# Fill matmuls in two more pauses of the routing, and another order on VectorE in the second-last expert tile

## The chip, the cores and the metric

One NeuronCore of a Trainium2 chip runs the whole program in one launch. The metric is the device time of one execution in microseconds; three runs of the kernel before gave 856.67, 857.29 and 859.13, with a median of 857.29.

## The reference

Three stages follow each other, all in float32.

- Attention with pooled queries: 16 heads (2 batches of 8) of 1152 keys and 64 columns; pairs of queries are averaged, so there are 576 queries for each head; softmax over the keys, product with the values. The result is laid out as x, 1152 tokens of 512 columns.
- A mixture of experts: x goes through two small products with w_gate and w_noise, from which noisy logits for 8 experts follow. Each token takes its best two experts, with softmax weights of these two, and gets the weighted sum of relu(x @ w1[e]) @ w2[e], with 1024 hidden columns.
- A dense layer: h = x @ w_in (2048 columns), g = h * cos(h), out = g @ w_out.

```python
logits = x @ w_gate
noisy_logits = logits + np.log1p(np.exp(x @ w_noise)) * noise
top2 = np.argpartition(-noisy_logits, 2, axis=1)[:, :2]
...
h = np.maximum(x[mask] @ w1[e], 0.0)
out[mask] += top2_w[mask, k, None] * (h @ w2[e])
...
h = x @ w_in
return (h * np.cos(h)) @ w_out
```

## The kernel before, in words

The program is written engine by engine: each engine has its own instruction stream, in the order of the code, and waits for semaphores that others raise. Nothing is scheduled by a planner. Large products are made of three matmuls in fp32r: each operand is split into a high part and a low part (the rest), and high x high, high x low and low x high are summed in PSUM (`split_product`, L1633 to L1635). So each operand needs a high half (a copy on ScalarE, `hh` in L862) and a low half (a subtraction on VectorE, `hl` in L1293, in `low_h`).

The attention runs to about 308 us. Its last step on TensorE is `turn_o` for the last head (L1470): ScalarE copies the head's output out of PSUM (L747, semaphore `ot_ev`), and TensorE turns it.

The routing follows, 308 to 326 us, with TensorE and VectorE in turns. VectorE makes noisy logits, the best two, and running counts by a scan (`upto`, L1113). TensorE makes ranks from them (`rank_of`, L1510 to L1514), and each expert's first tokens are picked by matmuls with a selection matrix (`first_tile`, L1527; once for each batch; VectorE makes the matrix `sel` in L1118 from `mine` in L1117). A table says which token stands in which slot (L1624, 20 matmuls of 26 columns); the gathers of x on GpSimd wait for it. `warm(n)` issues n matmuls of 512 columns on weights that lie in SBUF, into a PSUM bank that nobody reads (`IDLE`, bank 7; L1520). The kernel before calls it twice with WARM_R = 4: after the second ranks, and after the second `first_tile`. TensorE waits for `w_ready` (the weights of expert 0 are split) ahead of the second `rank_of`.

Then 25 expert tiles of 128 slots each. For tile t, TensorE turns the hidden values (`turn_h`, L1672), computes `hidden(t + 1)`, turns x for t + 2 (`turn_x`, L1648; not in the last tiles), and computes `expert_out(t)`, which waits for both low halves (`hl_ev` at 2t + 2). On VectorE, `tile_steps(t)` issues `low_h(t)`, `relu_d(t + 1)` (half of the ReLU, L1288), `low_x(t + 2)` and `move_y(t)` (L1300). `left` counts the tiles left after this one: in tile 23 `left` is 1, in tile 24 it is 0.

The first three token tiles of the dense layer are put together during the last two expert tiles. For slots of tiles up to 22, rows are gathered from DRAM by GpSimd, scaled by ScalarE (L886) and added by VectorE (`add_second`, L1307). For slots of tiles 23 and 24, `late_rows` (L1689) on TensorE multiplies the output tile by a selection matrix of gates, `late_sel`. VectorE prepares all this in `late_tiles()` at the start of tile 23: places and slot numbers (L1312 to L1319, semaphore `rt2_done`, for which GpSimd's gathers wait), and the gates (L1324 and L1327, for each of the two late tiles).

Of the kernel before, what the change touches and what calls it, by code (L numbers as in the profile page):

```python
# [10 lines left out]
ALU = mybir.AluOpType  # L11
# [4 lines left out]
P = 128  # L16
BANK = 512
# [25 lines left out]
WPIECES = 4  # L43
# [46 lines left out]
def bank_of(hh, slot):  # L90

    return 6 + (TURNS.index(slot) + hh) % 2
# [27 lines left out]
def build(nc, q, k, v, w_gate, w_noise, noise, w1, w2, w_in, w_out, out, x_rows, x_slots, y_slots, route):  # L120
    ctx = ExitStack()
    with ctx:
        def sem(name):
            return ctx.enter_context(nc.semaphore(name))
# [72 lines left out]
        w_ready = sem("w_ready")  # L197
# [53 lines left out]
        ps = ctx.enter_context(nc.psum_tensor("ps", [P, 8, BANK], F32))  # L251
        RANK0, RANK1, COUNTS, TABLE, IDLE = 7, 4, 5, 6, 7
# [15 lines left out]
        def place(name, at, shape, dt=F32):  # L268
            size = 4
            for n in shape[1:]:  # L270
                size *= n
            return nc.alloc_sbuf_tensor_at(name, shape, dt, offset=base + at), -(-(at + size) // 32) * 32


        W, at = place("W", 0, [P, 2, 2, 2 * DM * F // P], F32R)
# [26 lines left out]
        late_slot, at = place("late_slot", at, [P, 2])  # L302
# [96 lines left out]
        rtb, at = place("rtb", XD + 10240, [P, BLK, 4])  # L399
        late_sel, at = place("late_sel", at, [P, 2, BLK])  # L400
        assert at <= REGION + REGION_BYTES
        late_n, at = place("late_n", REGION + BLK_T * 2 * DM * 4, [P, 2, BLK])
# [576 lines left out]
        def _(dve):  # L979
            ve = nc.vector  # L980
            step_count = [0]

            def then(ins):

                step_count[0] += 1
                ins.then_inc(dve_step, 1)
                dve.wait_ge(dve_step, step_count[0])
# [246 lines left out]
            for n in range(2):  # L1234
                last = ve.tensor_tensor(based[:, n, :, :], onehot[:, n, :, :],
                                        tbase[:, :].unsqueeze(2).to_broadcast([P, E, RT]), ALU.mult)
            then(last)
            for n in range(2):
                last = ve.tensor_reduce(tile_of[:, n, :], based[:, n, :, :].rearrange("p e i -> p i e"), AX_X, ALU.add)
# [7 lines left out]
            last = ve.tensor_tensor(late[:, :, :], cum[0:1, 0:E - 1].unsqueeze(1).to_broadcast([1, SLOTS_T, E - 1]),  # L1247
                             iota_t[0:1, 0:SLOTS_T].unsqueeze(2).to_broadcast([1, SLOTS_T, E - 1]), ALU.is_le)
# [12 lines left out]
            def low_w(j):  # L1261

                dve.wait_ge(wh_done, WPIECES + j + 1)
                part = slice(j * WPIECE, (j + 1) * WPIECE)
                ve.tensor_tensor(W[:, 1, 1, part], stage[:, j % 2, :], W[:, 1, 0, part].bitcast(F32), ALU.subtract
                                 ).then_inc(w_ready, 1)

            def low_out(j):

                dve.wait_ge(oh_done, j + 1)  # L1270
                ve.tensor_tensor(W[:, 1, 1, j * WPIECE:(j + 1) * WPIECE], stage[:, j % 2, :],
                                 W[:, 1, 0, j * WPIECE:(j + 1) * WPIECE].bitcast(F32), ALU.subtract).then_inc(ol_done, 1)
# [9 lines left out]
            def low_x(t):  # L1282
                dve.wait_ge(xh_ev, t + 1)
                ve.tensor_tensor(xl[:, :, :], x_turned(t), xh[:, :, :].bitcast(F32), ALU.subtract).then_inc(xl_ev, 1)

            def relu_d(t):
                dve.wait_ge(h_done, 2 * t + 2)
                ve.tensor_scalar(hid[:, BANK:F], ps[:, 1, :], 0.0, None, ALU.max).then_inc(hid_d, 1)  # L1288

            def low_h(t):  # L1290
                for n in range(2):
                    dve.wait_ge(hh_ev, 2 * t + n + 1)
                    ve.tensor_tensor(hl[:, 4 * n:4 * n + 4, :].rearrange("p c n -> p (c n)"), ps[:, 2 + n, :],  # L1293
                                     hh[:, 4 * n:4 * n + 4, :].rearrange("p c n -> p (c n)").bitcast(F32),
                                     ALU.subtract).then_inc(hl_ev, 1)

            def move_y(t):
                dve.wait_ge(y_done, t + 2)
                at_least(dve, y_stored, 16 * t)
                ve.tensor_copy(ys[:, :], ps[:, 5, :]).then_inc(y_ev, 1)  # L1300

            def add_second(i):
                dve.wait_ge(xa_done, i + 1)
                dve.wait_ge(second_in[i % BLK_T], 16 * (i // BLK_T + 1))
                first = yg[:, i % BLK_T, 0, :]
                gate = gate_on[:, i, 1:2] if i < BLK_T else rt2[:, i, 3:4]
                ve.scalar_tensor_tensor(first, yg[:, i % BLK_T, 1, :], gate, first, ALU.mult, ALU.add).then_inc(x2_done, 1)  # L1307

            def late_tiles():

                dve.wait_ge(rt_loaded, 16)
                then(ve.scalar_tensor_tensor(pos_on[:, :, :], rt2[:, 0:BLK_T, 0:2], float(LATE * P), rt2[:, 0:BLK_T, 0:2],  # L1312
                                             ALU.is_lt, ALU.mult))
                ve.scalar_tensor_tensor(gate_on[:, :, :], rt2[:, 0:BLK_T, 0:2], float(LATE * P), rt2[:, 0:BLK_T, 2:4],
                                        ALU.is_lt, ALU.mult)
                ve.tensor_copy(pos2_u[:, BLK_T:TT, :], rt2[:, BLK_T:TT, 0:2])
                ve.tensor_copy(pos2_u[:, 0:BLK_T, :], pos_on[:, :, :]).then_inc(rt2_done, 1)
                for k in range(2):
                    last = ve.tensor_scalar(late_slot[:, k:k + 1], tok[:, 0:1], float((LATE + k) * P), None, ALU.add)  # L1319
                then(last)  # L1320
                dve.wait_ge(rtb_loaded, 16)
                for k in range(2):
                    for n in range(2):
                        last = ve.scalar_tensor_tensor(late_n[:, n, :], rtb[:, :, n], late_slot[:, k:k + 1], rtb[:, :, 2 + n],  # L1324
                                                       ALU.is_equal, ALU.mult)
                    then(last)
                    then(ve.tensor_tensor(late_sel[:, k, :], late_n[:, 0, :], late_n[:, 1, :], ALU.add))  # L1327

            def tile_steps(t, left=3, first=False):
                if left == 1:  # L1330
                    late_tiles()
                low_h(t)
                if left == 0:
                    add_second(1)
                    add_second(2)
                    low_out(0)
                    low_out(1)
                if first:
                    low_w(2)
                if left >= 1:  # L1340
                    relu_d(t + 1)
                if left == 1:
                    add_second(0)
                if first:
                    low_w(3)
                if left >= 2:
                    low_x(t + 2)
                move_y(t)
# [7 lines left out]
            relu_d(0)  # L1356
            low_x(1)
            tile_steps(0, first=True)
            with dve.Fori(1, SLOTS_T - 2) as t:
                tile_steps(t)  # L1360
            for left in (1, 0):
                tile_steps(SLOTS_T - 1 - left, left=left)
# [49 lines left out]
        def _(pe):  # L1412
# [53 lines left out]
            def turn_o(p, hh):  # L1466
                g = 2 * p + hh
                pe.wait_ge(ot_ev, g + 1)
                for c in range(QC):
                    last = pe.matmul(ps[:, bank_of(hh, ("o", 0)), c * TURN:(c + 1) * TURN], ot[0:D + 1, c * P:(c + 1) * P],  # L1470
                                     turner[:, bass.ds(g, 1), :].rearrange("p o n -> p (o n)"), start=True, stop=True)
                last.then_inc(ot_done, 1)
# [41 lines left out]
                    pe.matmul(ps[:, COUNTS, 0:E], ones[:, :], upto[:, :, RT - 1], start=True, stop=True  # L1514
                              ).then_inc(rank_done, 1)

            def warm(n):

                for i in range(n):
                    pe.matmul(ps[:, IDLE, :], W[:, 0, 0, 0:P], W[:, 0, 0, 0:BANK], start=True, stop=True)  # L1520

            def first_tile(b, sel):

# [58 lines left out]
            for c in range(QC):  # L1582

                at_least(pe, m0_ev, c - 1)
                for a in range(3):
                    last = pe.matmul(ps[:, 2 + c % 2 * 3 + a, 0:PIECE], qat[:, 0, c * P:(c + 1) * P],
                                     kt[:, 0, a * PIECE:(a + 1) * PIECE], start=True, stop=True)
# [20 lines left out]
            products(NHEAD // 2 - 1, 2, KC - 1)  # L1608
            pe.wait_ge(o_norm, NHEAD - 1)
            pe.wait_ge(rank_read, 1)  # L1610
            turn_o(NHEAD // 2 - 1, 1)


            first_tile(0, sel0)
            pe.wait_ge(w_ready, WPIECES)
            rank_of(1, RANK1)
            warm(WARM_R)
            first_tile(1, sel1)
            warm(WARM_R)
            pe.wait_ge(slot_of_done, 1)  # L1620
            pe.wait_ge(rows_done, 2)
            for n in range(2):
                for i in range(RT):
                    last = pe.matmul(ps[:, TABLE, 0:STW], row_of[:, n, i, :], tile_hot[:, n, i, :],  # L1624
                                     start=(n + i == 0), stop=(n * RT + i == 2 * RT - 1))
# [177 lines left out]
```

## Time and profile before

| | |
|---|---|
| three runs, us | 856.67, 857.29, 859.13 (median 857.29) |
| profiled execution, us | 856.61 |
| its span, from the first to the last instruction, us | 854.9 |
| TensorE (PE) busy | 838.0 us, 98% of the span |
| VectorE (DVE) busy | 499.9 us, 58% |
| ScalarE (ACT) busy | 421.9 us, 49% |
| GpSimd (POOL) busy | 402.1 us, 47% |
| mean granted TensorE clock | 0.998 |

The profiled execution's own time is 1.7 us over its span. PE's busy time goes by modelled ends of pipelined matmuls, so that the starts of instructions are the surer reading. A granted clock of 1.00 is 2.4 GHz, 0.50 is 1.2 GHz. "Idle before" is the time in which an engine stood, with the instruction that released it; "issue" stands where the profile shows no releaser.

### The profile page before, as it was taken

The page shows a single profiled execution, that of the slowest core. Times are in us where ns is not written, and L with a number is a line of the kernel's source. Part 1 is how long each engine was busy: PE and PEld are TensorE (multiplying, and loading weights), DVE is VectorE, ACT ScalarE, POOL GpSimd, SP SyncE. Part 2 cuts the span into 40 slices and gives each one's busy share as a digit, 9 for nine tenths or more (in the row PEclk, how much of TensorE's full clock was granted, in tenths as well). Part 3 has the DMA queues.
Part 4 walks back from the last instruction along what each step waited for, and adds up shares of the span by engine and source line. Part 5 has one row for each costly group of instructions (what it writes and reads, how often), then busy time and mean ns, then how long its engine had stood idle before and what let it go on. Part 6 is the DMA issues. An engine that isn't in the chain of part 4 may idle for free.

```text
span 854.9 us, 15389 instructions
## 1 busy us (share of the span) xinstructions
PE 838.0 (98%) x4860; PEld 744.4 (87%) x4861; DVE 499.9 (58%) x995; ACT 421.9 (49%) x776; POOL 402.1 (47%) x293
## 2 busy tenths in 40 slices
PE   7999999999999989999999999999999999999998
PEld 6899999999999887888887888888878889999897
DVE  7788877888778886423232322232266776676664
ACT  3777777777777763212111211121144665464554
POOL 7554445555877104649859959577422030000000
PEclk9999999999999999999999999999999999999999
DMA  5212211142242015986645545353444020000100
GB/s 132 66 43 62 64 41 41 41 141 73 94 128 95 1 56 188 305 307 224 236 155 176 193 146 184 130 201 133 137 130 154 1 74 19 20 0 1 38 1 37
DMA packets 51520, 91.27 MB, mean 107 GB/s; under 512 B 9376, under 2 KB 18592, under 8 KB 50976
## 3 DMA queue, kind: packets, MB, share of 16 engines
q1 hardware_dynamic: 40832, 67.26, 23.4%
q10 hardware_dynamic: 7296, 12.59, 4.5%
q0 software_dynamic: 3360, 11.01, 4.4%
q8 instruction: 18, 0.29, 0.1%
q14 instruction: 14, 0.11, 0.0%
HBM read 73.78 MB, written 17.06 MB: 106 GB/s over the span
## 4 chain that ended last, share of the span: by engine, by line
PE 90%; DVE 5%; ACT 2%; POOL 2%; issue 1%; DMA 0%; DVEq 0%; POOLq 0%; ACTq 0%
PE ps L1633 10%; PE ps L1635 10%; PE ps L1634 10%; PE ps L1455 5%; PE ps L1485 5%; PE ps L1501 4%; PE ps L1503 4%; PE ps L1502 4%; PE ps L1486 4%; PE ps L1760 4%; PE ps L1759 3%; PE ps L1758 3%; PE ps L1745 3%; PE ps L1743 3%; PE ps L1744 3%; PE ps L1672 2%
## 5 line engine op out<-in xcount | busy, mean ns | idle before, releaser
L639 POOL TENSOR_TENSOR W<-stage,W 128x2048 fp32r<-128x2048 f32 x32 | 147.1, 4598 | 2.6
L1023 DVE TENSOR_REDUCE mx<-ps 128x1 f32<-128x384 f32 x225 | 119.5, 550 | 17.3 <-PE ps L1455 17.3
L1035 DVE TENSOR_TENSOR pl__80<-ps,ph 128x576 fp32r<-128x576 f32 x144 | 107.9, 750 | 33.4 <-ACT ps L793 33.4
L788 ACT ACTIVATE ph<-ps 128x576 fp32r<-128x576 f32 x144 | 93.9, 652 | 53.5 <-PE ps L1486 52.5
L793 ACT ACTIVATE ps<-ps 128x576 f32<-128x576 f32 x144 | 93.4, 649 | 0.0
L862 ACT CAST hh<-ps 128x512 fp32r<-128x512 f32 x50 | 26.9, 590 | 124.2 <-PE ps L1672 113.5
L1501 PE MATMUL ps<-ph,vs 128*65 128x288 f32 x288 | 86.0, 299 | 0.4 <-ACT ot L747 0.4
L1485 PE MATMUL ps<-qat,kt 128*128 128x288 f32 x288 | 83.8, 306 | 1.3 <-DVE tok L1198 0.6
L1503 PE MATMUL ps<-ph,vs 128*65 128x288 f32 x288 | 84.7, 294 | 0.0
L1502 PE MATMUL ps<-pl__80,vs 128*65 128x288 f32 x288 | 84.6, 294 | 0.0
L1633 PE MATMUL ps<-W,xh 128*128 (+1 forms) x200 | 80.8, 404 | 1.0 <-POOL W L639 0.7
L1633 PE MATMUL ps<-W,hh 128*128 (+1 forms) x200 | 80.1, 401 | 1.3 <-issue 1.3
L1486 PE MATMUL ps<-qbt,k 128*128 128x288 f32 x288 | 80.3, 294 | 0.0
L1635 PE MATMUL ps<-W,xl 128*128 (+1 forms) x200 | 78.6, 393 | 0.0
L1634 PE MATMUL ps<-W,xh 128*128 (+1 forms) x200 | 78.5, 393 | 0.0
L1635 PE MATMUL ps<-W,hl 128*128 (+1 forms) x200 | 78.2, 391 | 0.0
L1634 PE MATMUL ps<-W,hh 128*128 (+1 forms) x200 | 78.0, 390 | 0.0
L1455 PE MATMUL ps<-kt,qat 128*128 128x384 f32 x225 | 76.1, 352 | 1.7 <-ACT qat L727 0.9
L1300 DVE COPY ys<-ps 128x512 f32<-128x512 f32 x25 | 17.3, 692 | 101.2 <-PE ps L1635 101.2
L1288 DVE TENSOR_SCALAR hid<-ps 128x512 f32<-128x512 f32 x25 | 17.3, 691 | 91.9 <-PE ps L1635 91.9
L1743 PE MATMUL ps<-fh,W 128*128 128x384 f32 x192 | 64.9, 338 | 0.0
L1745 PE MATMUL ps<-fh,W 128*128 128x384 f32 x192 | 64.8, 337 | 0.0
(220 smaller groups left out, 1959.3 us busy)
## 6 DMA issues: line engine op xcount, KB each, us to landing
stage<-in_moe_w_dram SPq DMA_DIRECT2D x32, 1024.0 KB, 5.5
y_slots<-ys ACTq DMA_DIRECT2D x25, 256.0 KB, 2.0
x_slots<-ring SPq DMA_DIRECT2D x22, 256.0 KB, 3.8
xs<-x_slots ACTq DMA_DIRECT2D x22, 256.0 KB, 2.7
kn<-in_k_dram SPq DMA_DIRECT2D x16, 288.0 KB, 3.4
vn<-in_v_dram SPq DMA_DIRECT2D x16, 288.0 KB, 2.9
stage<-in_moe_w_in_dram SPq DMA_DIRECT2D x4, 1024.0 KB, 5.0
stage<-in_moe_w_out_dram SPq DMA_DIRECT2D x4, 1024.0 KB, 5.7
```

Of the source, the lines that this page charges most:

```text
L639: pl.tensor_tensor(W[:, slot, 1, part], stage[:, j % 2, :], W[:, slot, 0, part].bitcast(F32), ALU.subtract).then_inc(w_ready, 1)
L1023: ve.tensor_reduce(mx3[:, i:i + 1], ps[:, bank_of(hh, ("m", i)), 0:PIECE], AX_X, ALU.max).then_inc(m_ev, 1)
L1035: ve.tensor_tensor(pl_[:, j % 3, :].rearrange("p (a n) -> p a n", a=2), ps[:, 2 * s_par(hh, j):2 * s_par(hh, j) + 2, 0:HQ], ph[:, j % 3, : ...
L1455: pe.matmul(ps[:, bank_of(hh, ("m", i)), 0:PIECE], qat[:, par, c * P:(c + 1) * P], kt[:, par, a * PIECE:(a + 1) * PIECE], start=True, stop ...
L1485: pe.matmul(ps[:, 2 * sp_ + a, 0:HQ], kt[:, par, keys], qat[:, par, cols], start=True, stop=False)
L1486: last = pe.matmul(ps[:, 2 * sp_ + a, 0:HQ], k1[:, par, keys], qbt[:, par, cols], start=False, stop=True)
L1501: pe.matmul(dst, vs[:, par, j, 0, :], ph[:, j % 3, cols], start=(j == 0), stop=False)
L1502: pe.matmul(dst, vs[:, par, j, 0, :], pl_[:, j % 3, cols], start=False, stop=False)
L1503: last = pe.matmul(dst, vs[:, par, j, 1, :], ph[:, j % 3, cols], start=False, stop=(j == KC - 1))
L1633: pe.matmul(dst, hi, rhs_of(i, 0), start=(i == 0), stop=False)
L1634: pe.matmul(dst, hi, rhs_of(i, 1), start=False, stop=False)
L1635: last = pe.matmul(dst, lo, rhs_of(i, 0), start=False, stop=(i == n - 1))
```

## The change

On VectorE, `late_tiles` becomes two functions, `late_places` and `late_gates(k)`. The places stay ahead of `low_h(23)`; the gates of the first late tile come behind `low_h(23)`, those of the second behind `relu_d(24)`. On TensorE, `warm` takes a bank, and is called twice more: three matmuls into bank 7 ahead of the last `turn_o`, and five into bank 5 behind the first `first_tile`. The wait for `w_ready` moves ahead of the first of them.

```diff
-            def late_tiles():
+            def late_places():
...
+            def late_gates(k):
+
                 dve.wait_ge(rtb_loaded, 16)
-                for k in range(2):
-                    for n in range(2):
-                        last = ve.scalar_tensor_tensor(late_n[:, n, :], rtb[:, :, n], late_slot[:, k:k + 1], rtb[:, :, 2 + n],
-                                                       ALU.is_equal, ALU.mult)
-                    then(last)
-                    then(ve.tensor_tensor(late_sel[:, k, :], late_n[:, 0, :], late_n[:, 1, :], ALU.add))
+                for n in range(2):
+                    last = ve.scalar_tensor_tensor(late_n[:, n, :], rtb[:, :, n], late_slot[:, k:k + 1], rtb[:, :, 2 + n],
+                                                   ALU.is_equal, ALU.mult)
+                then(last)
+                then(ve.tensor_tensor(late_sel[:, k, :], late_n[:, 0, :], late_n[:, 1, :], ALU.add))
 
             def tile_steps(t, left=3, first=False):
                 if left == 1:
-                    late_tiles()
+                    late_places()
                 low_h(t)
+                if left == 1:
+                    late_gates(0)
                 if left == 0:
                     add_second(1)
                     add_second(2)
@@
                 if left >= 1:
                     relu_d(t + 1)
                 if left == 1:
+                    late_gates(1)
                     add_second(0)
@@
-            def warm(n):
+            def warm(n, bank=IDLE):
 
                 for i in range(n):
-                    pe.matmul(ps[:, IDLE, :], W[:, 0, 0, 0:P], W[:, 0, 0, 0:BANK], start=True, stop=True)
+                    pe.matmul(ps[:, bank, :], W[:, 0, 0, 0:P], W[:, 0, 0, 0:BANK], start=True, stop=True)
@@
             pe.wait_ge(o_norm, NHEAD - 1)
             pe.wait_ge(rank_read, 1)
+            pe.wait_ge(w_ready, WPIECES)
+            warm(3, 7)
             turn_o(NHEAD // 2 - 1, 1)
 
 
             first_tile(0, sel0)
-            pe.wait_ge(w_ready, WPIECES)
+            warm(5, 5)
             rank_of(1, RANK1)
             warm(WARM_R)
             first_tile(1, sel1)
```

## Rows read from the trace of the kernel before

**Rows 1.** The page's chain of work that ended last, share of the span by engine.

```profile
PE 90%; DVE 5%; ACT 2%; POOL 2%; issue 1%; DMA 0%; DVEq 0%; POOLq 0%; ACTq 0%
```

**Rows 2.** Windows: length, busy us of each engine (instructions), granted clock, DMA, GB/s.

```profile
290.00:326.00 36.00, 32.94 (x253) 30.48 (x251) 28.62 (x126) 24.86 (x51) 0.00 (x0) 1.00 0.10 34
326.00:327.00 1.00, 1.00 (x7) 1.00 (x7) 0.26 (x3) 0.00 (x0) 0.00 (x0) 0.72 0.00 0
327.00:330.00 3.00, 3.00 (x9) 2.28 (x9) 2.93 (x6) 0.00 (x0) 2.48 (x2) 0.52 0.30 81
```

**Rows 3.** PE timeline, first hidden tile: start, us, line, tile, count [idle before <-releaser].

```profile
326.55 0.78 PE L1633 MATMUL ps<-W,xh 128*128 128x512 f32 x1
327.12 0.63 PE L1634 MATMUL ps<-W,xh 128*128 128x512 f32 x1
327.55 0.63 PE L1635 MATMUL ps<-W,xl 128*128 128x512 f32 x1
...
330.00 0.39 PE L1635 MATMUL ps<-W,xl 128*128 128x512 f32 x1
330.22 0.39 PE L1633 MATMUL ps<-W,xh 128*128 128x512 f32 x1
```

**Rows 4.** PE timeline, the routing.

```profile
308.05 0.29 PE L1503 MATMUL ps<-ph,vs 128*65 128x288 f32 x1
309.16 1.31 PE L1470 MATMUL ps<-turner,ot 65*128 65x81 f32 x10 [0.82 <-ACT ot L747]
310.31 4.67 PE L1527 MATMUL ps<-sel,x 128*128 128x128 f32 x40
316.15 0.39 PE L1510 MATMUL ps<-member,tri 128*128 128x40 f32 x2 [1.18 <-DVE upto L1113]
316.37 0.39 PE L1511 MATMUL ps<-upto,ones 128*128 128x40 f32 x2
...
316.82 1.18 PE L1520 MATMUL ps<-W 128*128 128x512 f32 x4
318.26 4.73 PE L1527 MATMUL ps<-sel,x 128*128 128x128 f32 x40 [0.27 <-DVE sel L1118]
...
324.27 2.44 PE L1624 MATMUL ps<-tile_hot,row_of 128*128 128x26 f32 x20 [0.35 <-ACT row_of L827]
```

**Rows 5.** Timelines of ScalarE, VectorE and GpSimd in the routing.

```profile
308.38 0.63 ACT L747 COPY ot<-ps 65x576 f32<-65x576 f32 x1 [2.26 <-PE ps L1503]
...
310.57 0.17 DVE L1046 TENSOR_SCALAR den_o<-ps 128x5 f32<-128x5 f32 x1 [0.31 <-DVE place_f L1134]
...
317.19 0.16 DVE L1117 SCALAR_TENSOR_TENSOR mine<-ps,member 128x5 f32<-128x5 f32 x1
...
327.22 1.12 POOL L673 DMA_INDIRECT xd<-x_rows,tok_u  x1 [46.95 <-DVE tok_u L1352]
```

**Rows 6.** ScalarE timeline, second high half of tile 23.

```profile
619.18 0.59 ACT L862 CAST hh<-ps 128x512 fp32r<-128x512 f32 x1
```

**Rows 7.** PE timeline, hidden(24), expert_out(23) and late_rows(0).

```profile
624.16 0.39 PE L1635 MATMUL ps<-W,xl 128*128 x1
625.87 0.50 PE L1633 MATMUL ps<-W,hh 128*128 x1 [1.31 <-issue]
...
632.38 2.85 PE L1689 MATMUL ps<-late_sel,ys 128*128 128x384 f32 x8
```

**Rows 8.** VectorE timeline, tile 23 and the start of tile 24.

```profile
619.62 1.71 DVE L1324 SCALAR_TENSOR_TENSOR late_n<-rtb,late_slot 128x384 f32<-128x384 f32 x2
621.37 0.56 DVE L1327 TENSOR_TENSOR late_sel<-late_n 128x384 f32<-128x384 f32 x1
...
624.31 1.29 DVE L1293 TENSOR_TENSOR hl<-ps,hh 128x512 fp32r<-128x512 f32 x2
625.51 0.68 DVE L1288 TENSOR_SCALAR hid<-ps 128x512 f32<-128x512 f32 x1
626.89 0.75 DVE L1307 SCALAR_TENSOR_TENSOR yg<-yg,gate_on 128x512 f32<-128x512 f32 x1 [0.69 <-DMA yg<-y_slots,pos_u]
631.63 0.69 DVE L1300 COPY ys<-ps 128x512 f32<-128x512 f32 x1 [3.99 <-PE ps L1635]
```

## The prediction

> **What bounds the kernel now.** I read the chain that ended last first: TensorE holds 90% of it and VectorE 5% [rows 1], so the end moves only by what TensorE itself is spared or made to wait. Then the granted clock by stretches: it is 1.00 over the whole routing (290 to 326 us), 0.72 in the microsecond after it, 0.52 in the next three. With a mean of 0.998 over 854.9 us (0.002 x 854.9 = 1.7 us of full clock missing, or 3.4 us at half) this is the one low stretch of the execution [rows 2]. Then TensorE's own timeline. At the low level (0.5 of full, so 1.2 GHz) one product of 512 columns follows another after 0.43 us, at the high level (2.4 GHz) after 0.23 us. From 326.55 to 330.00 us eight products are started in 3.45 us where 8 x 0.23 = 1.84 would do, so the low stretch costs 1.6 us [rows 3]. Last, TensorE's pauses. In the routing there are three small ones: 0.82 us before the turn of the last head (L1470), released by ScalarE's copy, 1.18 us before the ranks (L1510), released by VectorE's scan, and 0.3 us before the second selection [rows 4, 5]. In the last expert tiles there is one: the last product of hidden(24) starts at 624.16, the first of expert_out(23) only at 625.87, after 1.31 us of idle [rows 7]. The releaser is given as "issue", so I looked for it on VectorE. There the two low halves (L1293) of tile 23 run from 624.31 for 1.29 us, up to 625.60, directly before TensorE goes on; ScalarE's second high half had been there since 619.18 + 0.59 = 619.77 [rows 6, 8]. What stands before the low halves on VectorE are the gates of the two late tiles: two groups of 1.71 us and 0.56 us each. This wait is for hl_ev, and the gates make it.
>
> **Part 1, last expert tiles (VectorE).** Nothing is added or removed: four multiply-compares and two additions keep their forms. Before, the gates ran from 619.62 to about 624.27. After, the low halves start where the gates did or slightly earlier, limited by the high halves: the second is in at 619.77, so the low halves end by 619.8 + 1.29 = 621.1 at the latest. TensorE gets to expert_out(23) at 624.16 + 0.23 = 624.39, so 3.3 us of slack: the wait is gone. The idle time says 1.31 us; the starts say more, 625.87 - 624.39 = 1.48. The idle time goes by a modelled end of the last matmul, and the starts are what shifts the work behind them. I take 1.5 and keep 1.3 as the lower end.
>
> What is late next? Gates 0 (1.71 + 0.03 + 0.56 + 0.04 = 2.34 us) now stand ahead of the ReLU of tile 24 (L1288): 621.1 + 2.34 = 623.4, while the ReLU needs the end of hidden(24), 624.16 + 0.39 = 624.55. 1.1 us of cover. If that cover were gone, it would still cost nothing: the reader of the ReLU stands behind the 24 products of expert_out(23), 24 x 0.23 = 5.5 us. So the ReLU runs at 624.6 to 625.3, 0.9 earlier than its 625.51. Gates 1 then take up to 627.6, and the first add_second (L1307), at 626.89 now, moves to 627.6 and ends at 628.4. Behind it VectorE waits for the copy of tile 23's output, at 631.63 now and at 630.1 with the gain, 1.7 us later [rows 8]. The readers of the gates, late_rows at 632.38 now, come at 630.9, 3.3 us after gates 1 [rows 7]. The gathers are started from the places, which stay ahead of the low halves, so POOL's queue and its transfers keep their times. SP's queue is passed by nothing. All further work hangs on TensorE's chain and moves as a whole: -1.5 us.
>
> **Part 2, the two pauses (TensorE).** Added: 3 + 5 = 8 matmuls of 512 columns with their weight loads, into banks 7 and 5 whose old contents are read by then. The wait for the first weights (w_ready) moves ahead of the turn of the last head, with the fill, the turn and the whole selection queued behind it; but POOL has had nothing to do for 46.95 us before 327.22 us, so that all of its splits were done by 280.3 and this wait costs nothing [rows 5].
> Three in the first pause: TensorE's input is free at 308.05 + 0.13 = 308.18; the existing four take 1.18 us, so three take 1.18 - 0.23 = 0.95 with the last one's drain, 0.2 less until the input is free: 308.95. The turn starts at 309.16 now, being released by ScalarE's copy (308.38 + 0.63 = 309.01) [rows 4, 5]. Cost 0. Upper end: with the drain the fills reach to 308.2 + 0.95 = 309.15, and a wait's latency more makes the turn 0.1 late. Lower end -0.1, if an engine that streams starts the turn sooner than one that stood. This place has no cover: the turn heads VectorE's chain from 310.57 on.
> Five in the second: 1.18 + 0.23 = 1.41 with drain from 314.85, so 316.05 to 316.26 against 316.15 now; 0.1 late at most. The ranks (L1510, L1511, over at 316.37 + 0.39 = 316.76) have their reader, L1117 on VectorE, at 317.19, because VectorE still builds rows. 0.4 us of cover. Cost 0. If the cover were gone, it would be 0.1. The four fills and the second selection behind (318.26) have 0.27 us to spare [rows 4, 5].
> What does it bring? By the rows of this execution nothing fell in or after these pauses: the clock is 1.00 up to 326 us [rows 2]. What stands before the fall at about 326.5 is the table (L1624): 20 matmuls of 26 columns in 2.44 us, TensorE "busy" all along [rows 4]. The new fills lie 8 and 15 us earlier, with dense work, 4.7 us of selection and four fills, in between. I take 0 for the clock; the other end is -1.6, the whole low stretch gone. If it went, hidden(0) would end 1.6 us sooner, at 332.3; tile 1's gather, started at 327.22, has 5 us by then.
>
> The Trainium skill (TensorE: Matmul & The Clock Gate, "HAM oscillation — how this bites in real kernels") puts the fall of the clock down to long idle gaps between bursts of matmuls. Neither filled pause (0.8 and 1.2 us) is such a gap, and the trace agrees in that the clock stays at 1.00 through both; it disagrees in that the fall here follows an unbroken run of narrow matmuls. By the page the fills bring 0, as in my sum.
>
> **Sum.** Against the profiled execution: span 854.9, 1.7 around it, 856.61 in all; -1.5 + 0 + 0 = 855.1. The median of the runs before is 857.29, 0.7 above the profiled one, and the slowest, 859.13, is 2.5 above: about one low stretch more. I put the step on the median: 857.29 - 1.5 = 855.8.
>
> **Rivals.** A: *the low stretch goes.* For it: several pauses and narrow matmuls from 308 to 326 lie close together, and the fall may answer to this whole sparse stretch, not to the table alone; the spread of the runs suggests that stretches come and go between executions. Against: the table itself is untouched. 857.29 - 1.5 - 1.6 = 854.2.
> B: *the wait at 624 us is not hl's, or another comes as late.* For it: the profile names no releaser. Against: low halves and restart lie 0.26 us apart, and every other tile runs through without gap. -0.0: 857.3. Half of it would be 856.5.
> C: *slower.* The clock falls before the fills, in the pause at 308 us, and the fills run at 0.43 us each ahead of waiting work. Three take 1.3 us from 308.18: turn 0.35 late. The selection behind it loses up to 1.65 us of its pause of 1.18, 0.5 late; the five fills take 2.15 instead of 1.2, and the ranks twice their 0.6, which less the cover of 0.4 makes 1.0 late. In sum 1.85 against 1.5: 857.6. It decides from 1.5 us of delay. For it: the spread of the runs; against it: clock 1.00 there in the only trace.
> D: *the fills do more than the profiled execution can show*, since in the slower executions the clock falls after one of these pauses: the median comes down to the profiled one less 1.5, 855.1.
>
> **How the numbers follow.** Forecast (855.8, own range 855.2 to 856.6) 0.50; D 0.13; A 0.22; B 0.10; C 0.05. What a measurement of this kernel can tell from no change is about 0.3%, 2.6 us, so faster means under 854.7. That is A, and a tail of D and the forecast: 0.22 + 0.05 = 0.27. Slower means over 859.9: C at its worst, 0.03. The rest, 0.70, is within. Range: from just below A, 853.9, to B with the noise of the runs, 857.5.
>
> **What would show it.** Part 1 right: no idle before L1633 near 624 us, expert_out(23) starting 0.23 us after the last product of hidden(24), low halves done by 621.2, and the ReLU of tile 24 waiting for TensorE. Part 1 wrong: an idle time of over 0.3 us there, or a new one before L1672 or L1689. Part 2 right: fills end before 309.2 and 316.3, L1117 on VectorE not later against the turn, and the products of hidden(0) again 0.43 us apart for some 3 us. If they are 0.23 apart from the first on, A holds. If fills are 0.43 apart, C. A median under 854.7 or over 857.5 makes the prediction wrong.

## The result, and the profile after

The changed kernel has a median of 854.89 us (20 runs, 853.63 to 856.67); the kernel before, run beside it 20 times, 858.07. The ratio is 0.9965, 95% interval 0.9951 to 0.9978: 3.0 us less. A second set, run later with the last experiments (12 runs beside 23 of before), gave 0.9974 (0.9954 to 0.9994), 2.2 us less. The profiled execution took 854.54 us, its span is 852.8, 2.1 us under the one of before; its mean granted clock is 1.000, where it was 0.998.

The page's span, and the chain of work that ended last by engine. The chain has the same shape as before; TensorE's share is 89% where it was 90%:

```profile
span 852.8 us, 15404 instructions
PE 89%; DVE 5%; ACT 2%; issue 2%; POOL 2%; DMA 0%; DVEq 0%; POOLq 0%; ACTq 0%
```

The windows that answer to [rows 2]. The granted clock is the third figure from the end of a row:

```profile
290.00:326.00 36.00, 34.86 (x262) 31.85 (x260) 28.59 (x126) 24.71 (x50) 0.00 (x0) 1.00 0.10 34
326.00:327.00 1.00, 1.00 (x7) 0.91 (x7) 0.52 (x4) 0.00 (x0) 0.08 (x1) 1.00 0.00 0
327.00:330.00 3.00, 3.00 (x14) 2.44 (x13) 2.97 (x4) 0.60 (x1) 2.69 (x2) 1.00 0.30 87
```

The clock stays at 2.4 GHz where it had been at 1.2: 14 matmuls in the last window instead of 9. TensorE's timeline of the routing, for [rows 3 and 4] (L1475 is the turn, L1525 the fills, L1515 the ranks, L1631 the table, L1640 the first product of a group):

```profile
308.01 0.85 PE L1525 MATMUL ps<-W 128*128 128x512 f32 x3
308.90 1.34 PE L1475 MATMUL ps<-turner,ot 65*128 65x81 f32 x10
...
314.50 1.39 PE L1525 MATMUL ps<-W 128*128 128x512 f32 x5
315.83 0.42 PE L1515 MATMUL ps<-member,tri 128*128 128x40 f32 x2
...
324.04 2.37 PE L1631 MATMUL ps<-tile_hot,row_of 128*128 128x26 f32 x20 [0.35 <-ACT row_of L827]
326.26 0.48 PE L1640 MATMUL ps<-W,xh 128*128 128x512 f32 x1
326.58 0.39 PE L1641 MATMUL ps<-W,xh 128*128 128x512 f32 x1
```

And ScalarE's copy and the two places of VectorE, for [rows 5]:

```profile
308.21 0.64 ACT L747 COPY ot<-ps 65x576 f32<-65x576 f32 x1 [2.25 <-PE ps L1508]
...
310.34 0.17 DVE L1046 TENSOR_SCALAR den_o<-ps 128x5 f32<-128x5 f32 x1 [0.25 <-DVE place_f L1134]
...
316.96 0.16 DVE L1117 SCALAR_TENSOR_TENSOR mine<-ps,member 128x5 f32<-128x5 f32 x1
```

Both pauses are filled and neither chain waits: the turn starts 0.05 us after the copy (over at 308.21 + 0.64 = 308.85), where it was 0.15 before (309.01 to 309.16 [rows 4, 5]), and VectorE's L1117 starts 6.62 us after L1046, as before (317.19 - 310.57). From there to the table nothing moved either.

Tile 23 on TensorE and VectorE, for [rows 7 and 8] (gates are L1326 and L1329 now):

```profile
623.78 0.39 PE L1642 MATMUL ps<-W,xl 128*128 x1
624.01 0.39 PE L1640 MATMUL ps<-W,hh 128*128 x1
...
630.40 2.85 PE L1696 MATMUL ps<-late_sel,ys 128*128 128x384 f32 x8
```

```profile
619.21 1.29 DVE L1293 TENSOR_TENSOR hl<-ps,hh 128x512 fp32r<-128x512 f32 x2
620.42 1.72 DVE L1326 SCALAR_TENSOR_TENSOR late_n<-rtb,late_slot 128x384 f32<-128x384 f32 x2
622.17 0.56 DVE L1329 TENSOR_TENSOR late_sel<-late_n 128x384 f32<-128x384 f32 x1
624.28 0.69 DVE L1288 TENSOR_SCALAR hid<-ps 128x512 f32<-128x512 f32 x1 [1.55 <-PE ps L1642]
624.89 1.70 DVE L1326 SCALAR_TENSOR_TENSOR late_n<-rtb,late_slot 128x384 f32<-128x384 f32 x2
...
627.33 0.75 DVE L1307 SCALAR_TENSOR_TENSOR yg<-yg,gate_on 128x512 f32<-128x512 f32 x1
629.65 0.69 DVE L1300 COPY ys<-ps 128x512 f32<-128x512 f32 x1 [1.57 <-PE ps L1642]
```

The idle time is gone: the next group follows after 0.23 us. From the turns of tile 23 to those of tile 24 it is 11.80 us where it was 13.37.

**Where 2.1 us came from.** I followed the start of each tile's turns of the hidden values (L1672 before, L1679 after). hidden(0) starts 0.3 us earlier (326.26 for 326.55), 0.2 of it from ahead of the routing and 0.1 from the turn. Tile 0's turns start 1.83 us earlier (332.86 for 334.69): the low stretch is gone, worth 1.55. But tile 23's turns start only 0.41 us earlier (617.65 for 618.06). 1.4 us were given back on the way, 0.64 of them between tiles 1 and 2. VectorE and TensorE there, after:

```profile
343.94 2.29 DVE L1265 TENSOR_TENSOR W<-stage,W 128x2048 fp32r<-128x2048 f32 x1 [3.33 <-issue]
346.15 0.68 DVE L1284 TENSOR_TENSOR xl<-ps,xh 128x512 fp32r<-128x512 f32 x1
...
347.04 0.50 PE L1640 MATMUL ps<-W,xh 128*128 x1 [0.36 <-DVE xl L1284]
```

The last piece of expert 1's weights (L1265) is paced by its load, and it is queued ahead of the low half of x for tile 2 (L1284). Its high half on ScalarE waits for the transfer:

```profile
342.00 1.91 ACT L834 CAST W<-stage 128x2048 fp32r<-128x2048 f32 x1 [4.87 <-DMA stage<-in_moe_w_dram]
```

In the kernel before, this piece and the low half behind it came at the same times (343.82 and 346.03), and nobody waited, since TensorE itself was 1.8 us later. The rest, 0.8 us, comes from the pace of the tiles: 12.29 us each where it was 12.25, over 21 tiles. Here the turns of three tiles after the change (starts 12.30 and 12.29 apart):

```profile
383.12 1.03 PE L1679 MATMUL ps<-ident,hid 128*128 128x128 f32 x8
395.42 1.03 PE L1679 MATMUL ps<-ident,hid 128*128 128x128 f32 x8
407.71 1.03 PE L1679 MATMUL ps<-ident,hid 128*128 128x128 f32 x8
```

Then tile 23 adds 1.57. In sum 0.3 + 1.55 - 0.64 - 0.8 + 1.57 = 2.0, and 0.1 behind tile 24. The 0.8 us of the pace are not the change's doing, as the last section shows; without them this pair of profiles would lie 2.9 us apart.

### The profile page after: what moved, and what is told of

It is laid out like the page before. It is cut to its first block, busy times and chain, and to the rows that moved or that the text cites. A ratio compares the mean times of both kernels' runs of the same rounds, so it can differ in the third digit from the quotient of the medians.

```text
span 852.8 us, 15404 instructions
## 1 busy us (share of the span) xinstructions
PE 838.9 (98%) x4868; PEld 744.4 (87%) x4869; DVE 499.0 (59%) x995; ACT 422.2 (50%) x776; POOL 402.5 (47%) x293
## 4 chain that ended last, share of the span: by engine, by line
PE 89%; DVE 5%; ACT 2%; issue 2%; POOL 2%; DMA 0%; DVEq 0%; POOLq 0%; ACTq 0%
PE ps L1640 10%; PE ps L1642 10%; PE ps L1641 10%; PE ps L1460 5%; PE ps L1490 5%; PE ps L1506 4%; PE ps L1508 4%; PE ps L1507 4%; PE ps L1491 4%; PE ps L1766 4%; PE ps L1767 4%; PE ps L1765 4%; PE ps L1752 3%; PE ps L1750 3%; PE ps L1751 3%; PE ps L1679 2%
## 5 line engine op out<-in xcount | busy, mean ns | idle before, releaser
L1640 PE MATMUL ps<-W,xh 128*128 (+1 forms) x200 | 80.4, 402 | 1.3 <-POOL W L639 0.7
L1640 PE MATMUL ps<-W,hh 128*128 (+1 forms) x200 | 80.4, 402 | 0.0
```

The lines of the kernel that those rows point to most:

```text
L1640: pe.matmul(dst, hi, rhs_of(i, 0), start=(i == 0), stop=False)
```

## The experiments

Eleven runs: ten further kernels, and the changed one again. Medians differ from set to set, so each ratio is against the runs of the kernel before on the same chip, and each number of microseconds is worked out from the ratio. The mean granted clock of an execution tells how many low stretches it had behind its start: one of them takes it down by 0.002, as in [rows 2]. Over the three chips of the experiments the kernel before ran 90 times: 17 times without one, 48 times with one, 25 with two; by a line through these runs one stretch is worth 1.2 us. That is a rough figure: on the single chips the line gives 0.8, 1.2 and 1.6 us, and on the one of the wide table the few executions without a stretch were no faster than those with one (857.7 and 857.4 us on average). In the profiles a stretch in the start costs 1.2 to 1.4 us: from the turns of qb to the copy of the last head it is 293.3 to 293.5 us with it and 292.1 without. One at 326 us costs 1.55.

One thing the granted clock does not show is how long TensorE stays slow at the very start. The same six matmuls in the profile of before:

```profile
8.85 1.31 PE L1586 MATMUL ps<-kt,qat 128*128 128x384 f32 x6 [0.67 <-ACT qat L727]
```

And in the second profile of the changed kernel, with its window:

```profile
10.03 2.29 PE L1591 MATMUL ps<-kt,qat 128*128 128x384 f32 x6 [0.68 <-ACT qat L727]
...
8.00:12.00 4.00, 3.33 (x13) 2.92 (x12) 1.10 (x2) 1.51 (x4) 2.42 (x3) 1.00 0.81 178
```

In the second, they take 2.29 us for 1.31, and the slower pace lasts to about 15 us under a granted clock of 1.00; the last head's copy starts 2.6 us later (310.94 for 308.38). Over the thirteen profiles the turns of qb start anywhere from 16.0 to 18.9 us, and of all the edits only the fills of the start, in the last kernel, touch anything near them. So a time is more than its count of low stretches.

**Each edit alone, and each pause alone.** The order alone leaves both calls of the fills out, and the wait for `w_ready` is back in its old place (so too in each kernel below without the first fills):

```diff
-            warm(3, 7)
...
-            warm(5, 5)
```

> The new order on VectorE alone, no fills. Theory (each edit has its own share): 1.5 us of idle before expert_out(23) goes, nothing else, so about -1.5 against the kernel before (ratio 0.998), and low stretches of the clock in the routing as before. Rival (the order is all): ratio 0.9965 as with both edits. Rival (the fills are all): ratio 1.000.

Ratio 0.9983 (0.9972 to 0.9993), 1.46 us less; 1.1 low stretches an execution, as before. In its profile the stretch at 326 us is there, and the turns of tile 24 follow those of tile 23 after 11.78 us, where it was 13.37. This is the first theory's number.

The fills alone put both gates ahead of the low halves again:

```diff
                 if left == 1:
                     late_places()
+                    late_gates(0)
+                    late_gates(1)
                 low_h(t)
-                if left == 1:
-                    late_gates(0)
...
                 if left == 1:
-                    late_gates(1)
                     add_second(0)
```

> The fills alone, all gates ahead of the low halves again. Theory: the idle time of about 1.3 to 1.5 us before expert_out(23) is back, and what the two edits gave together beyond the order's share stays: about -1.3 (ratio 0.9985), since low stretches become fewer over the executions. Rival (the fills do nothing and the profiled execution was lucky): ratio 1.000, mean granted clocks as in the kernel before.

Ratio 0.9994 (0.9981 to 1.0007): 0.5 us less, unclear, and under the 1.3 that I expected. But the clock did move: 7 of 11 executions had no low stretch, where 5 of 33 of the kernel before on this chip had none; on average 0.36 for 1.1. The idle time is back:

```profile
628.09 0.50 PE L1639 MATMUL ps<-W,hh 128*128 x1 [1.28 <-issue]
```

Its profiled execution shows a second place where the clock falls, the start of the kernel; three other profiles show it too, the one with the fills of the first pause alone and the two with the wide table and no fills. This is the window in question:

```profile
24.00:26.00 2.00, 2.00 (x10) 1.86 (x9) 1.96 (x5) 1.19 (x2) 1.86 (x3) 0.50 0.03 8
```

Then one pause at a time, with the new order:

> Both edits less the five fills of the second pause: three fills ahead of the last turn_o stay. If the first pause matters for the clock and the second does not: as with both edits, ratio 0.9965. If it is the second that matters: as the order alone, 0.998. If they add up: 0.997 to 0.9975.

> Both edits less the three fills of the first pause: five fills ahead of the second ranks stay. If the second pause (1.18 us, the longer one) is what lets the clock fall: ratio 0.9965. If it is the first: as the order alone, 0.998. Either way the place costs nothing to TensorE's successors: L1117 on VectorE does not wait.

Three fills in the first pause: 0.9977 (0.9966 to 0.9988). Five in the second: 0.9984 (0.9973 to 0.9996). Neither can be told from the order alone by its time. By the clock they have 1.0 low stretch an execution each, with one execution of 11 without any, as the order alone. Both fills together gave the 0.36 above on the same chip. The changed kernel, with the same fills, has 0.7 over both its sets (11 of 32 without any), but in the second of them 0.75 beside 0.83 of the kernel before, 4 of 12 without any beside 9 of 23. So one fill alone did nothing that these runs can tell, both together helped clearly on one chip and not on another, and which of them saves which stretch is not settled.

**What lets the clock fall.** The table's matmuls have 26 columns, and I took them to be paced by their weight loads, so I let each stream its columns eight times:

```diff
-                    last = pe.matmul(ps[:, TABLE, 0:STW], row_of[:, n, i, :], tile_hot[:, n, i, :],
+                    last = pe.matmul(ps[:, TABLE, 0:WIDE * STW], row_of[:, n, i, :],
+                                     tile_hot[:, n, i, :].unsqueeze(1).to_broadcast([P, WIDE, STW]),
```

> Both edits, and each of the 20 matmuls of the table streams its 26 columns eight times (208 columns into the same bank, the first 26 are read), so the array has work behind each weight load. Theory (narrow matmuls of the table let the clock fall): no low stretch at 326 us in any execution, table still about 2.4 us since the weight loads pace it, hidden(0) at 0.23 us a product. Time against both edits: the stretch is worth 1.6 us on TensorE, of which 0.6 is given back at hidden(2), so where it had been, -1.0; over all executions about -0.4. Rival (the fall answers to the whole routing): the stretch stays in about half of the executions and the time is that of both edits, ratio 0.9965 to 0.998. Rival (208 columns cost time of their own): table over 2.6 us.

Ratio 0.9962 (0.9948 to 0.9977), by its time not to be told from the changed kernel. 9 of 12 executions had no low stretch, 0.25 on average; I had expected none in any. The table costs what it did, within 0.1 us, so its own columns do not pace it:

```profile
324.23 2.47 PE L1632 MATMUL ps<-tile_hot,row_of 128*128 128x208 f32 x20 [0.36 <-ACT row_of L828]
```

Its low half of x for tile 2 waits as after the change. The next kernel takes that wait away by an order on VectorE, and the same on ScalarE (`high_w(3)` behind `move_x`):

```diff
-                if first:
-                    low_w(3)
                 if left >= 2:
                     low_x(t + 2)
+                if first:
+                    low_w(3)
```

> As the run with the wide table, and in tile 0 the last piece of expert 1's weights (high part on ScalarE, low part on VectorE) comes behind the x of tile 2 on both engines. Theory: with the clock up, hidden(2) stands 0.4 to 0.6 us for the low half of x, which is queued behind this piece, and this wait goes: 0.4 to 0.6 us less than the wide table alone. Rival (the x of tile 2 is late for itself, by its gather): no change there.

Ratio 0.9956 (0.9941 to 0.9972), the lowest ratio of all; against the wide table alone 0.5 us less, within the intervals. The mechanism shows in the profile: the low half of x is 5.2 us earlier, the last weight piece comes behind it, and tile 2's turns follow tile 1's after 12.25 us instead of 12.89.

```profile
340.94 0.69 DVE L1286 TENSOR_TENSOR xl<-ps,xh 128x512 fp32r<-128x512 f32 x1 [0.36 <-ACT xh L851]
345.24 2.29 DVE L1267 TENSOR_TENSOR W<-stage,W 128x2048 fp32r<-128x2048 f32 x1 [3.61 <-ACT W L835]
```

The wide table in the kernel before, and with the other two but no fills:

> The kernel before with the wide table alone: no fills in the pauses, gates ahead of the low halves. Theory (the table is what lets the clock fall at 326 us): low stretch there gone, ratio 0.999, all else as before. If the pauses matter besides: some executions keep a low stretch. It also tells about the tile loop: products of a tile took 12.25 us from turn to turn where the execution had a low stretch at 326 us and 12.29 where it had none. If this follows the clock, it is 12.29 here; if it follows the fills of the first pause (the place of the loop in the code), 12.25.

> No fills in the two pauses; new order in tile 23, wide table, x of tile 2 ahead of the last weight piece. Theory: the fills are not needed once the table is wide; time as with both edits and these two (ratio 0.996). Rival (both fills keep the clock up besides): low stretches in a larger share of the executions and 0.5 to 1 us more than with the fills.

The table alone gave 0.9980 (0.9967 to 0.9993), 1.7 us less by the ratio, though the medians are only 0.8 apart (856.87 and 857.68). It has 0.33 low stretches an execution where the kernel before has 1.25 on this chip, and 8 of 12 executions without any for 3 of 34; this is what shows that the narrow table matters to the clock. Without the fills but with all else it was 0.9965 (0.9951 to 0.9978), with 0.36 low stretches; that is 0.8 us over the 0.9956 with the fills, but the intervals overlap, so what the fills bring beside the wide table is not decided. Both profiles have a low stretch that no other profile has, behind the unfilled second pause. Windows and selection of the kernel before with the wide table (clock third from the end):

```profile
319.00:323.00 4.00, 3.75 (x20) 3.62 (x20) 3.65 (x20) 3.01 (x6) 0.00 (x0) 0.57 0.00 0
```

```profile
317.28 0.39 PE L1511 MATMUL ps<-member,tri 128*128 128x40 f32 x2 [1.18 <-DVE upto L1114]
...
319.39 6.23 PE L1528 MATMUL ps<-sel,x 128*128 128x128 f32 x40 [0.25 <-DVE sel L1119]
```

The second selection takes 6.23 us for 4.73 [rows 4]. So the clock can fall behind this pause, and in the profiled execution of before it did not. Of the five profiles without fills in the second pause these two show it; of the seven with fills in both pauses none does. That speaks for the pause as the cause, but so few profiles do not show it, and both also had a stretch in the start.

**The costs of the fills.** Both doubled, `warm(6, 7)` and `warm(10, 5)`:

> Both fills doubled: six ahead of the last turn_o, ten behind the first selection. It tests the costs of the sum. Theory: three and five just fit. Three more cost 3 x 0.23 = 0.7 us at turn_o, with no cover. Five more end 1.15 us later; the ranks then end 0.75 us after L1117 on VectorE could start, as the cover is 0.4. In sum the table comes about 1.4 us later than with both edits. Rival (the fills are hidden further, since VectorE and ScalarE set the pace of the routing): table later by under 0.5 us.

A single execution, for its profile (856.85 us; its start was slow, with the turns of qb at 18.19 us for 16.11, so this time says nothing on the fills):

```profile
310.08 1.53 PE L1525 MATMUL ps<-W 128*128 128x512 f32 x6
311.45 1.24 PE L1475 MATMUL ps<-turner,ot 65*128 65x81 f32 x10
...
316.95 2.55 PE L1525 MATMUL ps<-W 128*128 128x512 f32 x10
319.34 0.31 PE L1515 MATMUL ps<-member,tri 128*128 128x40 f32 x2
```

```profile
319.90 0.16 DVE L1117 SCALAR_TENSOR_TENSOR mine<-ps,member 128x5 f32<-128x5 f32 x1 [0.41 <-PE ps L1516]
```

The turn starts 0.53 us after the copy (310.92) instead of 0.05, and L1117 waits 0.41 us. From the copy to the table 16.1 us instead of 15.2: 0.9 us in all, between my 1.4 and the rival's 0.5. The sizes three and five fit; doubled, the first makes the turn 0.5 us later and the second makes L1117 wait 0.4.

**The changed kernel again, and the start.** The last kernel adds to the one with the wide table and x first

```diff
             qb_group(0, 0, 1)
+            warm_up(WARM_S)
...
+                                if early and hh == 1 and i == 0:
+                                    warm_up(WARM_S + 2)
                                 max_scores(p, hh, i)
```

where `warm_up(n)` issues n matmuls of 384 columns into bank 5, and WARM_S is 3.

> Both edits, wide table, x of tile 2 first, and fills of 384 columns in two pauses of the start as well: three before the first scores of head 0 (pause of 0.6 us), five before the first maxima of head 1 (pause of 0.9 us). Theory (a low stretch falls where pauses crowd, and one such place is 16 to 24 us): the stretch seen at 23.6 us in two of the profiles goes, mean clock near 1.000, and the median 0.3 to 0.5 us under the version without these fills. Rival (fills in the start delay the scores or maxima): first turn_o later by 0.2 us or more, and nothing won.

> The changed kernel once more, beside the others on one chip. As a yardstick: ratio 0.9965 to 0.9975, about two thirds of a low stretch an execution, and the version with the wide table and x first 0.5 to 1 us under it. Its tile pace may be 12.25 or 12.29 us: if it is 12.25 here, the pace belongs to the execution and not to the kernel.

On one chip: the changed kernel 855.18 us (0.9974, 0.9954 to 0.9994), with 0.75 low stretches; the one with all of it 853.94 (0.9960, 0.9944 to 0.9976), and 11 of 12 executions without any. Its median is the lowest of all, but its ratio is not (0.9956 without the fills of the start, on another chip, with 8 of 12 executions without a stretch). The two were not run side by side, so what these fills add is not shown. They fit the first pause: the scores start 1.56 us after the turns of qb (16.91 to 18.47), as in the kernel before (16.31 to 17.87).

```profile
17.62 0.77 PE L1533 MATMUL ps<-kt,qat 128*128 128x384 f32 x3
18.47 0.37 PE L1493 MATMUL ps<-qat,kt 128*128 128x288 f32 x1
...
19.44 1.12 PE L1533 MATMUL ps<-kt,qat 128*128 128x384 f32 x5
20.53 0.62 PE L1463 MATMUL ps<-kt,qat 128*128 128x384 f32 x2
```

And the pace: the same changed kernel, which had 12.29 us a tile in its first profile, has 12.26 and 12.25 here. The low stretch behind the table is there again in this profile:

```profile
386.80 1.03 PE L1679 MATMUL ps<-ident,hid 128*128 128x128 f32 x8
399.06 1.03 PE L1679 MATMUL ps<-ident,hid 128*128 128x128 f32 x8
411.31 0.93 PE L1679 MATMUL ps<-ident,hid 128*128 128x128 f32 x7
```

## Why the prediction was right, and where not

The time, 854.89 us, lies in the stated range (853.9 to 857.5), but not in the forecast's own (855.2 to 856.6), and is nearest to rival D's 855.1. The step was forecast as 1.5 us and measured as 3.0 and 2.2. So the range held by its rivals, and only the first part of the sum held by its mechanism.

**Part 1 was right in place and size.** 1.5 us was forecast; the profile gives 1.57 (13.37 less 11.80), the order alone 1.46 by its ratio. The wait was hl_ev's. The low halves ended at 620.50 (forecast 621.1), the ReLU started at 624.28 (624.6) with TensorE as its releaser, gates 1 ended at 627.18 (627.6), and none of the moved work made anyone wait. The fills alone brought the idle time back. Rival B is out.

**Part 2 was right in its costs, wrong in what it brings.** Cost 0, with bounds of 0.1 on either side: the turn starts 0.1 us sooner after the copy, the lower end. The term that was mis-sized is the clock's. The step that failed is "by the rows of this execution nothing fell in or after these pauses", from which I took 0. It is true of that execution and was no ground for the median: the clock's falls differ between executions of one kernel, and a profile shows one. The kernel before had 1.1 low stretches an execution (0.8 to 1.25 by chip). Its own profile shows one behind the table; two more places, the start and behind the second pause, are seen in profiles of kernels that have its code there. The changed one has 0.7. At 1.2 us a stretch that is 0.5 us, as an estimate; in the changed kernel's second set it is 0.75 beside 0.83, or 0.1 us. By times, the share of the fills is 0.5 us alone (interval to 1.6 less and 0.6 more), and both edits less the order alone gives 3.0 - 1.5 = 1.5 in one set and 2.2 - 1.5 = 0.8 in the other. So 0.5 to 1.5 at face value, and the interval of the fills alone takes in none at all: the order's 1.5 us is shown, and that the fewer stretches make up the rest is likely and not shown.

**Rivals A and D are each half of what happened.** In the profiled execution the low stretch at 326 us was gone, as in A, and TensorE won 1.55 us (forecast 1.6). But only 7 of the 20 executions had a mean clock of 1.000, so this profile was a lucky draw, and the stretch stayed in the second profile of the changed kernel. The fills don't remove it; at best they make falls rarer over the executions, as D has it. What A missed is that the gain doesn't reach the end: 0.64 us go to the wait for the low half of x. I had checked the gather of tile 1 as the thing that is late next, and not the weight piece that stands ahead of x in VectorE's queue. C did not happen: its condition, a fall of the clock in the pause at 308 us, is in no profile. With fills doubled the table was 0.9 us late at the full clock, so larger fills do cost.

The Trainium skill (TensorE: Matmul & The Clock Gate, "HAM oscillation — how this bites in real kernels") speaks of waits between bursts. The runs agree in part: behind the second pause (1.18 us) the clock was seen to fall only where it was not filled, in two profiles of five. They go beyond it in the table: TensorE was busy throughout, and giving its matmuls more columns took the falls from 1.25 to 0.33 an execution on one chip.

## What to carry to other kernels

Look at granted clocks of many executions before pricing a fill: one profile shows one draw, and the mean clock beside each time tells how often it falls behind the start, though not how long the start itself is slow. Where a stretch of narrow matmuls does not get longer with more columns, let them stream more: it cost under 0.1 us, it took most low stretches away, and alone it gave 1.7 us by the ratio (0.6 to 2.8). And where TensorE gets faster in one stage, check each queue ahead of its next operand, not only the transfer for it.

## What the runs showed that I had not expected

Two paces of the same expert tile, 12.25 and 12.29 us, constant over an execution from tile 2 on, but for one step of 13.3 us that every profile has; over the whole loop 0.9 us. In the slow one the first ten products after the turns follow each other after 0.231 us on average, in the other only the first three after 0.232, and all behind them after 0.227; that makes 0.03 of the 0.04 us. It could be tied to the fills of the first pause or to the clock at 326 us. Neither holds: the kernel before with the wide table has no fills and 12.29, and the changed kernel had both paces in two executions. It belongs to the execution; its cause is open.
